# A second value product per head pair in three half passes, a copy moved to GpSimd and a subtraction moved ahead of a row maximum

## What is computed

```python
q_rot, k_rot = (rotate(q), rotate(k))
scores = scale * np.matmul(q_rot, k_rot.transpose(0, 1, 3, 2))
scores = scores - np.max(scores, axis=-1, keepdims=True)
attn = np.exp(scores)
attn = attn / (np.sum(attn, axis=-1, keepdims=True) + 1e-09)
x = np.matmul(attn, v).astype(np.float32)     # then to (tokens, heads * columns)
h = x @ w_in
e = np.exp(h - h_max)
sm = e / (np.sum(e, axis=-1, keepdims=True) + 1e-09)
solu = h * sm
ln = (solu - mu) / np.sqrt(var + 1e-06) * g_ln
out = ln @ w_out
```

## Time and profile before

| | |
|---|---|
| median of three runs | 487.47 us |
| profiled execution | 487.08 us |
| its span | 485.3 us |
| TensorE busy | 476.8 us, 98% |
| VectorE busy | 368.7 us, 76% |
| ScalarE busy | 264.4 us, 54% |
| GpSimd busy | 191.9 us, 40% |

### The profile page before, as it was taken

One profiled execution on the slowest core, in us unless ns is written; L12 is line 12 of the kernel. 1 busy time (PEld: TensorE's weight loads), 2 busy tenths in 40 slices (PEclk: granted clock), 3 DMA queues, 4 the chain that ended last, 5 costly groups with the idle time before them and its releaser, 6 DMA issues.

```text
span 485.3 us, 7697 instructions
## 1 busy us (share of the span) xinstructions
PE 476.8 (98%) x2527; PEld 403.1 (83%) x2527; DVE 368.7 (76%) x580; ACT 264.4 (54%) x397; POOL 191.9 (40%) x238
## 2 busy tenths in 40 slices
PE   8899999999999999999999999999999999999997
PEld 7677888988888888888888878888888888888885
DVE  6869787787778777877876356999897899888731
ACT  4667787778788778877787353033224222322221
POOL 6856356536453654565361012343343121122110
PEclk9999999999999999999999999999999999999999
DMA  8503454535454554445424112133333233322332
GB/s 291 188 12 76 138 158 110 178 123 162 117 156 143 144 148 141 155 108 166 149 72 99 39 34 52 32 65 87 81 70 86 47 54 67 80 56 60 62 77 85
DMA packets 101007, 50.58 MB, mean 104 GB/s; under 512 B 90280, under 2 KB 90280, under 8 KB 99048
## 3 DMA queue, kind: packets, MB, share of 16 engines
q1 hardware_dynamic: 100152, 50.00, 38.3%
q10 hardware_dynamic: 816, 0.10, 0.1%
HBM read 33.33 MB, written 4.79 MB: 79 GB/s over the span
## 4 chain that ended last, share of the span: by engine, by line
PE 95%; DVE 2%; ACT 1%; DMA 1%; POOL 1%; issue 0%; SPq 0%; DVEq 0%; POOLq 0%; ACTq 0%
PE ps L1087 22%; PE ps L1101 20%; PE ps L1115 20%; PE ps L1039 18%; PE ps L1010 8%; PE ps L1054 4%; PE ps L1067 2%; DMA X<-x_in 1%; POOL xT L394 1%; DVE nm L782 1%; DVE X L723 1%; DVE X L728 0%; ACT QK L541 0%; ACT p_main L593 0%; ACT QK L556 0%
## 5 line engine op out<-in xcount | busy, mean ns | idle before, releaser
L782 DVE TENSOR_REDUCE nm<-ps 128x1 fp32r<-128x576 f32 x144 | 108.2, 756 | 49.7 <-PE ps L1010 47.4
L1087 PE MATMUL ps<-p_main,V 128*128 128x288 f32 x456 | 129.5, 406 | 0.0
L593 ACT ACTIVATE p_main<-ps 128x576 f32<-128x576 f32 x114 | 74.2, 651 | 39.5 <-PE ps L1039 37.2
L1039 PE MATMUL ps<-QK 128*128 128x288 f32 x320 | 92.9, 371 | 0.8 <-ACT p_main L593 0.5
L394 POOL TENSOR_TENSOR X<-X,rope 128x1152 f32<-128x1152 f32 x26 | 68.7, 2665 | 59.9 <-DVE KB L767 59.7
L1101 PE MATMUL ps<-w_hi,KB 128*128 128x512 f32 x288 | 91.4, 390 | 0.0
L1115 PE MATMUL ps<-w_hi,QK 128*128 128x512 f32 x288 | 90.8, 389 | 0.0
L1087 PEld LDWEIGHTS ps<-p_main,V 128*128 128x128 f32 x456 | 80.3, 190 | 12.2 <-ACT p_main L593 0.2
L1039 PEld LDWEIGHTS ps<-QK 128*128 128x128 f32 x320 | 56.7, 189 | 19.3 <-issue 5.7
L1039 PE MATMUL ps<-KB 128*128 128x288 f32 x320 | 67.7, 293 | 0.0
L614 ACT ACTIVATE X<-ps,neg_max 128x1024 f32<-128x1024 f32 x18 | 20.1, 1119 | 83.3 <-DVE neg_max L827 83.3
(11 more groups left out here) (101 smaller groups left out, 646.8 us busy)
## 6 DMA issues: line engine op xcount, KB each, us to landing
X<-x_in SPq DMA_DIRECT2D x13, 1152.0 KB, 5.2
V<-oe SPq DMA_DIRECT2D x213, 32.0 KB, 1.9
V<-v_in SPq DMA_DIRECT2D x32, 160.0 KB, 2.7
out<-X SPq DMA_DIRECT2D x18, 256.0 KB, 2.3
w_raw<-w_in SPq DMA_DIRECT2D x16, 256.0 KB, 2.9
xT<-x_in SPq DMA_DIRECT2D x2, 1152.0 KB, 10.3
xT<-oe SPq DMA_DIRECT2D x16, 144.0 KB, 2.4
inv<-inv_rows SPq DMA_DIRECT2D x16, 144.0 KB, 2.9
```

The lines of the kernel that those rows point to most:

```text
L593: nc.scalar.activation(dst[:, :].rearrange("p (b c) -> p b c", b=2), score_ps[:, :, 0:HALF], ACT.Exp, scale=SCALE).then_inc(exp_done, 1)
L782: nc.vector.tensor_reduce(nm[g][:, at:at + 1], src[:, :, 0:HALF], AX_XY, ALU.max, negate=True)\
L1039: ins = nc.tensor.matmul(score_ps[:, half, 0:HALF], keys[:, of:of + P], queries[:, to + half * HALF:to + (half + 1) * HALF], start=(g == 0 ...
L1087: ins = nc.tensor.matmul(o_ps[a][:, half, 0:HALF], v, p[:, half * HALF:(half + 1) * HALF], start=(k == 0), stop=(k == 9))
```

## The change

`HALVED` becomes `(3, 8)`: in pairs 1 to 14 head B's third full product, k = 8 in step 8, is made of halves too. There are now two sets of `v_hi` and `v_lo`, one `p_hi` and one `p_lo`. For k = 8 the exponentials of step 7 go to `o_ps[0]`. The second copies of head A's queries for pairs 3 to 15 are made by GpSimd, behind `rotate` and `add`, with a semaphore of their own; pair 2's stays with ScalarE. GpSimd's `set_tails` and head A's `halve_v` now stand ahead of `divide`, head B's behind it. `low_keys(n + 2, 0)` moves from step 7, behind `row_max(n + 1, 7)`, to step 6, ahead of it; `low_p(n, 1)` takes the place in step 7. ScalarE's `high` is renamed `set_high`. The core of the diff:

```diff
-HALVED = 3
+HALVED = (3, 8)
...
+            def second_queries(m):
+
+                pool.wait_ge(score_ready, STEPS * (m - 2) + BOTH + 1)
+                nc.gpsimd.tensor_copy(QK[m % 2][other(0), 0, 0:S], x_of(m)[own(0), 1, :]).then_inc(second_done, 1)
+                pool.wait_ge(second_done, m - 2)
...
-            halve_v(1)
+            halve_v(1, 0)
+            halve_v(1, 1)
...
+                if n + 2 < PAIRS:
+                    pool.wait_ge(rot_done, n + 3)
+                    second_queries(n + 2)
+                    set_tails(n + 2)
+                if halved(n + 1, HALVED[0]):
+                    halve_v(n + 1, 0)
                 if n >= 2:
-                    if n + 2 < PAIRS:
-                        pool.wait_ge(rot_done, n + 3)
                     divide(n - 2)
-                if n + 2 < PAIRS:
-                    set_tails(n + 2)
-                if halved(n + 1, HALVED):
-                    halve_v(n + 1)
+                if halved(n + 1, HALVED[1]):
+                    halve_v(n + 1, 1)
...
-                if s < BOTH and halved(n, s):
-                    act.wait_ge(o_taken, 2 * n)
-                    nc.scalar.activation(o_ps[1][:, :, 0:HALF], score_ps[:, :, 0:HALF], ACT.Exp, scale=SCALE)\
+                if s != BOTH and halved(n, s + s // BOTH):
+                    a = s // BOTH
+                    act.wait_ge(o_taken, 2 * n + a)
+                    nc.scalar.activation(o_ps[1 - a][:, :, 0:HALF], score_ps[:, :, 0:HALF], ACT.Exp, scale=SCALE)\
...
-                    if s == (8 if n == 0 else 7) and n + 2 < PAIRS:
-                        second_queries(n + 2, 0)
+                    if n == 0 and s == 8:
+                        second_queries(2, 0)
...
-                    if s == 3 and halved(n, HALVED):
-                        low_p(n)
+                    if s == 3 and halved(n, HALVED[0]):
+                        low_p(n, 0)
+                    if s == 7 and halved(n, HALVED[1]):
+                        low_p(n, 1)
...
-                    if s == 7 and n + 2 < PAIRS:
+                    if s == 6 and n + 2 < PAIRS:
                         low_keys(n + 2, 0)
...
+                    if m >= 3:
+                        pe.wait_ge(second_done, m - 2)
...
+            def weigh_halves(n, a):
+
+                pe.wait_ge(v_lo_done[a], n)
+                pe.wait_ge(p_hi_done, halves(n, a))
+                pe.wait_ge(p_lo_done, halves(n, a))
+                for v, p in ((v_hi[a], p_hi), (v_lo[a], p_hi), (v_hi[a], p_lo)):
```

More of the change, by code:

```diff
@@ L89, in attention_then_mlp @@
         p_lo = sb("p_lo", [P, S], F32R)
-        v_hi = sb("v_hi", [P, P], F32R)
-        v_lo = sb("v_lo", [P, P], F32R)
+        v_hi = [sb(f"v_hi_{h}", [P, P], F32R) for h in "ab"]
+        v_lo = [sb(f"v_lo_{h}", [P, P], F32R) for h in "ab"]
         oe = [sb(f"oe{c}", [P, 2, S]) for c in range(2)]
@@ L104, in attention_then_mlp @@
         p_lo_done = sem("p_lo_done")
-        v_hi_done = sem("v_hi_done")
-        v_lo_done = sem("v_lo_done")
+        v_hi_done = [sem(f"v_hi_{h}_done") for h in "ab"]
+        v_lo_done = [sem(f"v_lo_{h}_done") for h in "ab"]
+        second_done = sem("second_done")
         x_loaded = [sem(f"x_loaded{c}") for c in range(2)]
@@ L216, in halved, with halves, high, copied @@
         def halved(n, k):
-            return k == HALVED and 1 <= n < PAIRS - 1
+            return k in HALVED and 1 <= n < PAIRS - 1
+        def halves(n, a):
+            return 2 * (n - 1) + a + 1
+        def high(m, a):
+            return m + 4 if a == 0 and m >= 3 else 2 * m + 1
+        def copied(m, a):
+            return m + 4 if a == 0 and m >= 3 else 2 * m + 2
         def last_pair(t):
@@ L259, in wait_x @@
                 for a in range(2):
[L260 removed]
+                    sp.wait_ge(hi_done[a], copied(m - 2, a))
                     sp.wait_ge(low_k_done[a], m - 1)
@@ L264, in wait_x @@
                     sp.wait_ge(tails_set, 3 * (m - 2))
+                if m >= 5:
+                    sp.wait_ge(second_done, m - 4)
             def load_x(m):
@@ L417, in set_tails, with halve_v @@
                 pool.wait_ge(tails_set, 3 * m)
-            def halve_v(m):
+            def halve_v(m, a):
                 pool.wait_ge(v_loaded[m % 2], uses(m) * 32)
                 if m >= 2:
[L423 to L429, removed]
+                    pool.wait_ge(pv_done, PVS * (m - 1) + HALVED[a] + 1)
+                    pool.wait_ge(v_lo_done[a], m - 1)
+                v = V[m % 2][:, a, (HALVED[1] - 5 if a else HALVED[0] + 1), own(a)]
+                nc.gpsimd.tensor_copy(v_hi[a][:, own(a)], v).then_inc(v_hi_done[a], 1)
+                pool.wait_ge(v_hi_done[a], m)
+                nc.gpsimd.tensor_tensor(v_lo[a][:, own(a)], v, v_hi[a][:, own(a)].bitcast(F32), ALU.subtract)\
+                  .then_inc(v_lo_done[a], 1)
+                pool.wait_ge(v_lo_done[a], m)
+            def second_queries(m):
+                pool.wait_ge(score_ready, STEPS * (m - 2) + BOTH + 1)
+                nc.gpsimd.tensor_copy(QK[m % 2][other(0), 0, 0:S], x_of(m)[own(0), 1, :]).then_inc(second_done, 1)
+                pool.wait_ge(second_done, m - 2)
             def divide(m):
@@ L465, in _ @@
                 nc.gpsimd.memset(V[c][:, 1, :, 0:D], 1.0).then_inc(v_const, 1)
-            nc.gpsimd.memset(v_hi[:, D:P].bitcast(F32), 1.0).then_inc(v_const, 1)
-            nc.gpsimd.memset(v_lo[:, D:P].bitcast(F32), 0.0).then_inc(v_const, 1)
-            pool.wait_ge(v_const, 6)
+            for a in range(2):
+                nc.gpsimd.memset(v_hi[a][:, other(a)].bitcast(F32), 1.0).then_inc(v_const, 1)
+                nc.gpsimd.memset(v_lo[a][:, other(a)].bitcast(F32), 0.0).then_inc(v_const, 1)
+            pool.wait_ge(v_const, 8)
             nc.gpsimd.memset(expo[:, :], -0.5).then_inc(const_done, 1)
@@ L535, in _, with set_high @@
         def _(act):
-            def high(m, a):
+            def set_high(m, a):
                 c, at = m % 2, COLS[a]
@@ L584, in exp @@
                         act.wait_ge(pv_done, PVS * was + (i + 1 if i < 4 else i + 3))
-                if s < BOTH and halved(n, s):
-                    act.wait_ge(o_taken, 2 * n)
-                    nc.scalar.activation(o_ps[1][:, :, 0:HALF], score_ps[:, :, 0:HALF], ACT.Exp, scale=SCALE)\
+                if s != BOTH and halved(n, s + s // BOTH):
+                    a = s // BOTH
+                    act.wait_ge(o_taken, 2 * n + a)
+                    nc.scalar.activation(o_ps[1 - a][:, :, 0:HALF], score_ps[:, :, 0:HALF], ACT.Exp, scale=SCALE)\
                       .then_inc(exp_done, 1)
                     act.wait_ge(exp_done, STEPS * n + s + 1)
-                    nc.scalar.activation(p_hi[:, :].rearrange("p (b c) -> p b c", b=2), o_ps[1][:, :, 0:HALF], ACT.Copy)\
-                      .then_inc(p_hi_done, 1)
+                    nc.scalar.activation(p_hi[:, :].rearrange("p (b c) -> p b c", b=2), o_ps[1 - a][:, :, 0:HALF],
+                                         ACT.Copy).then_inc(p_hi_done, 1)
                     return
@@ L648, in _ @@
                 if 2 <= n < PAIRS - 1:
-                    high(n + 1, 1)
+                    set_high(n + 1, 1)
                 for s in range(STEPS):
@@ L652, in _ @@
                     if n == 1 and s == 0:
-                        high(2, 1)
+                        set_high(2, 1)
                     if n == 1 and s == 1:
@@ L657, in _ @@
                         if s == 2:
-                            high(1, 0)
+                            set_high(1, 0)
                             second_queries(1, 0)
                         if s == 3:
-                            high(1, 1)
+                            set_high(1, 1)
                         if s == 4:
@@ L688, in _ @@
                     if s == (7 if n == 0 else 6) and n + 2 < PAIRS:
-                        high(n + 2, 0)
-                    if s == (8 if n == 0 else 7) and n + 2 < PAIRS:
-                        second_queries(n + 2, 0)
+                        set_high(n + 2, 0)
+                    if n == 0 and s == 8:
+                        second_queries(2, 0)
             take_o(PAIRS - 1, 1)
@@ L790, in row_max, with low_p @@
                     nc.vector.transpose(nm_row[g][:, :], nm[g][:, :].bitcast(F32)).then_inc(turned[g], 1)
-            def low_p(n):
-                dve.wait_ge(p_hi_done, n)
-                nc.vector.tensor_tensor(p_lo[:, :].rearrange("p (b c) -> p b c", b=2), o_ps[1][:, :, 0:HALF],
+            def low_p(n, a):
+                dve.wait_ge(p_hi_done, halves(n, a))
+                nc.vector.tensor_tensor(p_lo[:, :].rearrange("p (b c) -> p b c", b=2), o_ps[1 - a][:, :, 0:HALF],
                                         p_hi[:, :].bitcast(F32).rearrange("p (b c) -> p b c", b=2), ALU.subtract)\
@@ L992, in row_scores @@
                 if i == BOTH:
-                    pe.wait_ge(hi_done[1], 2 * m + 2)
+                    pe.wait_ge(hi_done[1], copied(m, 1))
```

(6 more changed lines are left out.)

8 lines of the change are left out of this document (4 added, 4 removed).

## The result

The changed kernel takes 493.68 us (median of 4 runs, 493.66 to 493.83), the kernel before on the same chip 487.49: a ratio of 1.0126 with a 95% interval of 1.0113 to 1.0138. It is 6.2 us slower; 5.5 were forecast, as 493.0 us.

What follows compares the result with a forecast made beforehand. TensorE, busy 98% of the span, bounds the kernel. Pairs 2 to 13 add 4.6 us, pair 14 0.25, pair 1 0.7: +5.5 on 487.08 gives 492.6, plus 0.4 for the median, 493.0 us; range 490.0 to 496.4.

Steps and rivals of the forecast that it cites:

- The saving: Step 8's product in halves instead of float32: 0.17 us less TensorE work a pair, 2.4 us over 14 pairs.
- The wait: TensorE in step 8 waits for p_lo: bare chain 0.41 us late, low_p ending at 153.25, TensorE starting at 153.30.
- the forecast of 0.38 a pair: Pairs 2 to 13 each get 0.38 us longer, with the 0.17 us saved already in it; together 4.6 us.
- the signs I named: Changed profile: TensorE idle 0.45 to 0.6 us before step 8's six matmuls, pairs about 17.0 us, maximum 0.47 later.
- The early low keys: Low keys ahead of step 7's maximum cost step 8's row_scores 0.1 us at most, inside the p_lo wait.
- Rival A: GpSimd's copies and VectorE's low keys contend: 0.23 us more in each of 13 pairs, 496.0 us; chance 0.16.
- Pair 1: First halved pair: 0.38 us longer, plus 0.3 for GpSimd's second split ahead of rotate(3), together 0.7 us.
- My either-or for `w_low`: w_low beside the later rotate(3) slips in, winning up to 1.0 us, or waits for its second instruction, losing 0.7.
- Pair 14: No low keys here, so the bare chain ends 0.13 us sooner and the pair gets 0.25 us longer.
- B: Operands ready when TensorE reaches step 8's product: 0.17 us won in 14 pairs, about 485.1 us; chance 0.09.

Runs made afterwards that it cites:

- the last run: Changed kernel with p_lo's wait before the fifth matmul, halve_v(1, 1) behind rotate(3), and pair 1's low keys between step 7's maximum and low_p: 486.49 us.

## Why the prediction was right, step by step

**The saving.** I had 0.17 us for three passes. Between the run with one halved product and the one with two and a late wait, pairs differ by 16.75 - 16.55 = 0.20. Nearly all of it lies between the two score matmuls by KB around the product: over pairs 2 to 13 that stretch is 1.86 us with the float32 product and 1.68 with the six (means of the two runs). So the product saves 0.18 to 0.20 and not 0.17: my price came from step 4, where product and score matmuls take 1.06 us, and in step 8 they take 1.03 to 1.06. By the four passes of which the page "FP8 and Floating Point Precision" of the Trainium skill (TensorE Precision Notes) speaks, the estimate was 0.24 us; the runs stay below it.

**The wait.** Right in mechanism and place. The chain of exponential, copy and subtraction, the low keys in front of the maximum, the overlap of the maximum with what follows: `low_p` was to start 1.41 to 1.53 us behind the exponential, and starts 1.43 behind it. That the forecast of 0.38 a pair met 0.37 so closely is in part luck: three sizes were off and cancel. `low_p` ended 0.06 us sooner than I took, and TensorE came 0.14 us behind it (156.56 to 156.70), not 0.05; from there to the score matmuls by KB it took 1.12 us, not 1.16. Of the signs I named, the pairs of 17.0 us, the low keys right behind `set_high` and the maximum of step 7 0.48 us later in the pair came; TensorE's recorded idle time is 0.22 us and not 0.45 to 0.6, for the reason given with the page. Seen by parts, as the runs give them: early low keys +0.09, three passes -0.20, the wait at the front +0.48, together +0.37.

**The early low keys.** I wrote that `row_scores` of step 8 loses 0.1 us at most and that it lies inside the wait for `p_lo`. In the changed kernel both hold, but the loss is one of its own: it stays when the wait is gone, and 12 x 0.09 = 1.1 us is what it takes from the version with the late wait.

**GpSimd.** Rival A, contention that makes the low keys long, is out: they took 0.75 us in each of pairs 2 to 13. In pair 7 they started within 0.01 us of a cast of GpSimd, at 154.35, and the cast took 0.85 us instead of 0.23. GpSimd paid. The copy's return to ScalarE changed nothing. The rule of the page "GPSIMD Engine Reference" of the Trainium skill (Specifications) says that Vector instructions with two SBUF inputs contend with GpSimd, and the trace agrees, with either engine paying. The run with the low keys late shows the dear case: low keys of 1.17 us behind a division that had begun, while the division kept its 1.42. There the one that came later got long; so it was in the kernel before, where the cast to `v_hi` at 152.22 took 0.70 us beside low keys from 152.07.

**Pair 1.** This was the wrong term, and most of the 0.7 us between 493.0 and 493.68. I had +0.7 (0.3 more than another pair), it is +1.26 (0.89 more). The late `rotate(3)` costs 0.49, measured by undoing it, against my 0.3. I did not see that in this pair `set_high(3, 0)` comes so late that the early low keys cost 0.41 and not 0.09 (18.38 against 17.97, with one product halved). My either-or for `w_low` was too short: it slipped in, which was the branch that was to win up to 1.0, and the later and longer `rotate` held up `add` instead.

**Pair 14 and the rest.** From pair 14's halved product of step 4 to the end the changed kernel takes 0.24 us more (268.00 to 491.5, and 262.04 to 485.3). I had 0.25, for pair 14 alone, and that agreement is luck too: pair 14's step 8 is 0.32 us longer (from its halved product of step 4 to the score matmul by KB behind step 8's product 8.98 us against 8.66), and 0.08 us are lost again somewhere behind it. The start up to the first one is 0.22 us longer (44.37 against 44.15); in the other kernels it varies from 44.30 to 44.79 us, so I can't assign it. Summed: 0.22 + 1.26 + 4.48 + 0.24 = 6.2.

**The rivals.** B, operands in time, gave 485.1. With the late wait they are in time where they are used, and the kernel is at 487.3, or 486.3 with `rotate(3)` first, since the early low keys and pair 1 keep 1 to 2 us of it.

## What to carry to other kernels

Before trading one operand for two halves, count from the start of the chain that makes the last half to the first instruction that waits, and compare it with a place where the same trade works: here the cover was 0.53 us shorter, against 0.13 us to spare in the other place, and that made the wait. Wait for an operand where it is first used, not where the group that uses it begins. When an engine without slack has a wait removed or added, look at each queue the new instruction stands in, since what is behind it (a maximum, a rotation) hands the delay on somewhere else.

## What the runs showed that I had not expected

TensorE started 0.14 us after `low_p` had ended, in the changed kernel and in the run with the late low keys (159.77 to 159.92, 0.15), but 0.05 after a maximum (153.65 to 153.70). The first has three semaphores to wait for and a producer with 576 columns a partition to write, the second one semaphore and one column; the rows above decide between the two. The same `low_p` with one semaphore waited for (pair 1 of the last run) ended at 54.28, and the matmul started at 54.33, 0.05 later. The maximum in the run with the low keys late ended at 161.76, and `row_scores` of the next pair's step 0, which waits for five semaphores, started at 161.91, 0.15 later, and 0.14 or 0.15 later in each of pairs 2 to 13 of that run. So the lag goes with the number of semaphores waited for, one or several, and not with what the producer writes.

A wait that ends just as TensorE arrives still costs 0.09 us, with the weight load starting only with its matmul: two float32r matmuls took 0.36 and not 0.27 us in pair 7 of the run with one halved product, and 11 of its pairs 2 to 13 are 0.08 to 0.09 us longer than before.
